# Fused attention and two gated feed-forward layers on one Trainium2 core: fill-in products of zeros, and another order of the GpSimd, SyncE and weight-sum work

## What is computed

```python
q_d, k_d, v_d = (a.reshape(B, H, S // 4, 4, D).mean(axis=3) for a in (q, k, v))
out_up = np.repeat(softmax_attention(q_d, k_d, v_d), 4, axis=2)   # averages of four positions
mask = np.abs(pos[:, None] - pos[None, :]) < 4                     # the band
scores = np.where(mask, scale * q @ k.T, -1e9)
attn_out = out_up + softmax(scores) @ v
x = attn_out.transpose(0, 2, 1, 3).reshape(B * S, H * D)
x = gated(x, w_in, w_out, 1.0);  x = gated(x, w_in2, w_out2, 1.702)
# gated: h = x @ w_in; (h * sigmoid(c * h)) @ w_out
```

## Time and profile before

| | |
|---|---|
| time, median of 3 runs (lowest, highest) | 829.08 us (828.62, 831.41) |
| time of the profiled execution | 831.32 us |
| its span, first to last instruction | 829.4 us |
| mean granted TensorE clock | 0.994 of full speed |
| attention, from the start to the last addition into `x` | about 121.8 us of the span |
| busy: PE, PEld, DVE, ACT, POOL | 806.5, 778.4, 653.4, 536.2, 191.8 us |

### The profile page before, as it was taken

How to read it: one execution, slowest core, us unless ns; L and a number is a source line. 1 busy time by engine, 2 the same in 40 slices (tenths; PEclk the granted TensorE clock), 3 DMA queues, 4 the chain that set the end, 5 groups by cost and what they waited for, 6 DMA issues and landing times.

```text
span 829.4 us, 15638 instructions
## 1 busy us (share of the span) xinstructions
PE 806.5 (97%) x5787; PEld 778.4 (94%) x5787; DVE 653.4 (79%) x945; ACT 536.2 (65%) x865; POOL 191.8 (23%) x191
## 2 busy tenths in 40 slices
PE   7988899999999999999999999999999999999998
PEld 4766679999999999999999999999999999999997
DVE  6889869989989867888767888899756677665465
ACT  5887775667735567745677555687465787365763
POOL 6678768612025511036300000000000000000000
PEclk8999999999999999999999999999999999999999
DMA  7878756877677897768887787877887777878773
GB/s 211 246 196 231 200 163 234 276 245 260 205 247 249 274 311 263 251 209 262 265 288 254 232 258 251 271 244 235 301 282 260 265 252 265 290 241 267 270 260 126
DMA packets 98315, 205.42 MB, mean 248 GB/s; under 512 B 8416, under 2 KB 56032, under 8 KB 98240
## 3 DMA queue, kind: packets, MB, share of 16 engines
q1 hardware_dynamic: 98240, 204.42, 75.5%
HBM read 160.87 MB, written 43.52 MB: 246 GB/s over the span
## 4 chain that ended last, share of the span: by engine, by line
PE 76%; DVE 8%; DMA 6%; issue 3%; POOL 3%; ACT 2%; SPq 0%; DVEq 0%; POOLq 0%; ACTq 0%
PE hid L322 39%; PE yp L345 35%; DMA vn<-in_v 5%; DVE gr L498 2%; POOL vpair L897 2%; DMA wr<-in_w_in 1%; DVE wh L294 1%; DVE xs L255 1%; PE pt L1090 1%; ACT xs L251 1%; ACT wh L285 0%; DVE x L1063 0%; ACT yt L938 0%; POOL pband L900 0%; ACT pavg L988 0%
## 5 line engine op out<-in xcount | busy, mean ns | idle before, releaser
L322 PE MATMUL hid<-xs,wh 128*128 128x384 f32 x2016 | 352.9, 335 | 3.2 <-DVE hw L478 2.1
L322 PEld LDWEIGHTS hid<-xs,wh 128*128 128x128 f32 x2016 | 349.0, 188 | 6.1 <-issue 4.8
L345 PE MATMUL yp<-gr,wh 128*128 128x384 f32 x2016 | 352.5, 335 | 1.8 <-DVE gr L498 1.8
L345 PEld LDWEIGHTS yp<-gr,wh 128*128 128x128 f32 x2016 | 351.0, 189 | 2.3 <-issue 2.3
L285 ACT ACTIVATE wh<-wr 128x1024 fp32r<-128x1024 f32 (+1 forms) x164 | 164.5, 1003 | 157.7 <-PE hid L322 118.0
L498 DVE TENSOR_TENSOR gr<-G,gr 128x768 fp32r<-128x768 f32 x144 | 138.6, 971 | 48.3 <-ACT gr L398 48.2
L398 ACT ACTIVATE gr<-G 128x768 fp32r<-128x768 f32 x144 | 121.8, 846 | 68.9 <-PE yp L345 67.6
L294 DVE TENSOR_TENSOR wh<-wr,wh 128x1024 fp32r<-128x1024 f32 x76 | 89.4, 1176 | 23.1 <-ACT wh L285 23.0
L365 ACT ACTIVATE G<-G 128x1152 f32<-128x1152 f32 x48 | 55.8, 1162 | 0.0
L488 DVE TENSOR_TENSOR G<-hv,hid 128x384 f32<-128x384 f32 x48 | 26.5, 552 | 27.0 <-PE hid L322 26.9
L473 DVE TENSOR_TENSOR hv<-p,hid 128x384 f32<-128x384 f32 x48 | 26.4, 549 | 26.9 <-PE hid L322 19.3
(11 more groups left out here) (94 smaller groups left out, 766.8 us busy)
## 6 DMA issues: line engine op xcount, KB each, us to landing
wh<-rests SPq DMA_DIRECT2D x72, 512.0 KB, 3.8
wr<-sums_out SPq DMA_DIRECT2D x48, 512.0 KB, 4.7
wr<-in_w_out SPq DMA_DIRECT2D x36, 512.0 KB, 5.2
rests<-wh SPq DMA_DIRECT2D x36, 512.0 KB, 3.3
wr<-sums_in SPq DMA_DIRECT2D x40, 384.0 KB, 4.0
wr<-in_w_in SPq DMA_DIRECT2D x40, 256.0 KB, 3.4
qk<-in_qkT SPq DMA_DIRECT2D x11, 576.0 KB, 6.3
G<-in_w_in SPq DMA_DIRECT2D x12, 512.0 KB, 7.2
```

The lines of the kernel that those rows point to most:

```text
L322: last = eng.matmul(hid[:, at, 0:HALF], lhsT=wh[:, w % SLOTS, part, a % 4, cc * P:(cc + 1) * P], rhs=xs[:, rest, q, cc, :], start=start an ...
L345: last = eng.matmul(yp[:, at + m, 0:HALF], lhsT=wh[:, w % SLOTS, part, p % 4, m * P:(m + 1) * P], rhs=gr[:, p, rest, :], start=start and p ...
```

## The change

A 16-bit tile `zeros` is added. VectorE clears it as its first instruction, and the 11 warm-up products of TensorE now read it and wait only for that (`zero`); the wait for the mask and `ident16` moves behind them. The same helper, `keep_warm`, runs seven more products of zeros (128x128 by 128x512, 16 bits) into the transposes' PSUM banks in the body of unit 0, after `avg_scores(0)`, and six in the body of unit 1, after `band_scores(1)`.

GpSimd builds the mask before the two identities. In each unit it scales the band weights first, then makes `vpair`, then `vavg` (of which there are now two), then the weight sums. The sums of block p come one unit later than before: two in the odd unit 2p+1, two in the even unit 2p+2 (the last block has all four in unit 15).

SyncE loads q and k for u+3 first, then waits for `v_half` and loads `vn`, then the v windows, and in even units the block of `G` that the next unit uses. The first block is loaded after `vn` of unit 1 and q and k of unit 3.

```diff
+    IDLE = (7, 6)
+            zeros = sb("zeros", [P, P], BF16)
-            vavg = sb("vavg", [P, 2, 2 * D])
+            vavg = [sb(f"vavg{i}", [P, 2, 2 * D]) for i in range(2)]
 # SyncE
             def body(u, first=False):
-                if u.n + 1 < UNITS:
-                    eng.wait_ge(v_half, u.n + 1)
-                    load_vn(u.after())
                 if u.n + 3 < UNITS:
...
                     load_qk(u.after().after().after())
                 if u.n + 1 < UNITS:
+                    eng.wait_ge(v_half, u.n + 1)
+                    load_vn(u.after())
                     if not first:
                         eng.wait_ge(band_out, u.n)
                         load_vwin(u.after())
-                if u.odd and u.n + 1 < UNITS:
-                    eng.wait_ge(ffn.w0_sum, 2 * u.n)
-                    ffn.first_raw(eng, u.half + 1)
+                if not u.odd:
+                    if u.half:
+                        eng.wait_ge(ffn.w0_sum, 4 * u.half - 2)
+                    ffn.first_raw(eng, u.half)
             start(Unit(0, 0))
-            ffn.first_raw(eng, 0)
 # GpSimd
             eng.wait_ge(consts_fill, 3)
-            identity(ident16)
-            eng.wait_ge(consts, 1)
             fills = 3
...
             eng.sem_inc(consts, 1)
+            identity(ident16)
+            eng.wait_ge(consts, 2)
             identity(ident)
...
+                eng.wait_ge(b_rcp, u.n + 1)
+                e = pband[u.odd]
+                eng.tensor_tensor(e[:, :, 0:WIN], e[:, :, 0:WIN], rcb[:].unsqueeze(2).broadcast_to([P, NT, WIN]),
+                                  ALU.mult).then_inc(b_nrm, 1)
                 eng.wait_ge(vn_in, DMA_INC * (u.n + 1))
                 if not first:
                     eng.wait_ge(v_sum, u.n)
                 rows = vn.rearrange("p j (r d) -> p r j d", r=FACTOR)
                 eng.tensor_tensor(vpair[:], rows[:, 0:2], rows[:, 2:4], ALU.add).then_inc(v_half, 1)
-                eng.wait_ge(b_rcp, u.n + 1)
-                e = pband[u.odd]
-                eng.tensor_tensor(e[:, :, 0:WIN], e[:, :, 0:WIN], rcb[:].unsqueeze(2).broadcast_to([P, NT, WIN]),
-                                  ALU.mult).then_inc(b_nrm, 1)
                 eng.wait_ge(v_half, u.n + 1)
+                if u.n > 1:
+                    eng.wait_ge(avg_out, u.n - 1)
+                eng.tensor_tensor(vavg[u.odd][0:HP], vpair[:, 0], vpair[:, 1], ALU.add).then_inc(v_sum, 1)
                 if not first:
-                    eng.wait_ge(avg_out, u.n)
-                eng.tensor_tensor(vavg[0:HP], vpair[:, 0], vpair[:, 1], ALU.add).then_inc(v_sum, 1)
-                sum_weights(u)
+                    sum_weights(u)
             def sum_weights(u):
+                p = (u.n - 1) // 2
...
                 if u.odd:
+                    eng.wait_ge(ffn.w0_in, DMA_INC * (p + 1))
                     eng.tensor_tensor(at(S1), at(A21), at(A22), ALU.add).then_inc(ffn.w0_sum, 1)
                     eng.tensor_tensor(at(S3), at(A11), at(A21), ALU.subtract).then_inc(ffn.w0_sum, 1)
+                if not u.odd or u.n + 1 == UNITS:
...
 # VectorE
-            for pad in (vwin[P // 2:], vavg[P // 2:]):
+            eng.memset(zeros[:], 0.0).then_inc(zero, 1)
+            for pad in (vwin[P // 2:], vavg[0][P // 2:], vavg[1][P // 2:]):
                 eng.memset(pad, 0.0).then_inc(pads, 1)
 # TensorE
                     band_scores(u)
+                if u.n == 1:
+                    keep_warm(IDLE[1], pt)
...
                     avg_scores(u)
                 if first:
+                    keep_warm(IDLE[0], pt)
                     eng.wait_ge(consts, 3)
...
-            eng.wait_ge(consts, 1)
-            for n in range(WARM):
-                eng.matmul(sa if n % 2 else sc[:, 0, :], lhsT=ident16[:], rhs=ident16[:].unsqueeze(1).broadcast_to(
-                    [P, 4, P]), start=True, stop=True)
+            def keep_warm(times, to):
+                for n in range(times):
+                    eng.matmul(to[n % 2], lhsT=zeros[:], rhs=zeros[:].unsqueeze(1).broadcast_to([P, 4, P]),
+                               start=True, stop=True)
+            eng.wait_ge(zero, 1)
+            keep_warm(WARM, (sc[:, 0, :], sa))
+            eng.wait_ge(consts, 2)
             eng.wait_ge(band_cp, 2)
-            eng.wait_ge(pads, 5)
+            eng.wait_ge(pads, 6)
```

More of the change, by code:

```diff
@@ L769, in build @@
             OA = 640
+        zero = sem("zero")
         consts = sem("consts")
@@ L867, in identity @@
                                   pattern=[[-1, P]], channel_multiplier=1).then_inc(consts, 1)
+            eng.memset(band[:, 0:3, :], 0.0).then_inc(consts_fill, 1)
             eng.memset(ident16[:], 0.0).then_inc(consts_fill, 1)
-            eng.memset(band[:, 0:3, :], 0.0).then_inc(consts_fill, 1)
             eng.memset(ident[:], 0.0).then_inc(consts_fill, 1)
             eng.wait_ge(consts_fill, 3)
-            identity(ident16)
-            eng.wait_ge(consts, 1)
             fills = 3
@@ L897, in body @@
                 eng.tensor_tensor(vpair[:], rows[:, 0:2], rows[:, 2:4], ALU.add).then_inc(v_half, 1)
-                eng.wait_ge(b_rcp, u.n + 1)
-                e = pband[u.odd]
-                eng.tensor_tensor(e[:, :, 0:WIN], e[:, :, 0:WIN], rcb[:].unsqueeze(2).broadcast_to([P, NT, WIN]),
-                                  ALU.mult).then_inc(b_nrm, 1)
                 eng.wait_ge(v_half, u.n + 1)
+                if u.n > 1:
+                    eng.wait_ge(avg_out, u.n - 1)
+                eng.tensor_tensor(vavg[u.odd][0:HP], vpair[:, 0], vpair[:, 1], ALU.add).then_inc(v_sum, 1)
                 if not first:
-                    eng.wait_ge(avg_out, u.n)
-                eng.tensor_tensor(vavg[0:HP], vpair[:, 0], vpair[:, 1], ALU.add).then_inc(v_sum, 1)
-                sum_weights(u)
+                    sum_weights(u)
             def sum_weights(u):
+                p = (u.n - 1) // 2
                 def at(a):
-                    return ffn.first_place(u.half, a)
+                    return ffn.first_place(p, a)
                 if u.odd:
[L914 to L919, removed]
+                    eng.wait_ge(ffn.w0_in, DMA_INC * (p + 1))
                     eng.tensor_tensor(at(S1), at(A21), at(A22), ALU.add).then_inc(ffn.w0_sum, 1)
                     eng.tensor_tensor(at(S3), at(A11), at(A21), ALU.subtract).then_inc(ffn.w0_sum, 1)
+                if not u.odd or u.n + 1 == UNITS:
+                    eng.wait_ge(ffn.w0_sum, 4 * p + 2)
+                    eng.tensor_tensor(at(S2), at(S1), at(A11), ALU.subtract).then_inc(ffn.w0_sum, 1)
+                    eng.wait_ge(ffn.w0_sum, 4 * p + 3)
+                    eng.tensor_tensor(at(S4), at(A12), at(S2), ALU.subtract).then_inc(ffn.w0_sum, 1)
             for n, pad in enumerate((ptb[P // 2:], pta[P // 2:])):
@@ L999, in early @@
                     ffn.round_x(eng, 0, FILLS[n - 7])
-            eng.wait_ge(consts, 2)
+            eng.wait_ge(consts, 1)
             eng.activation(band[:, NT - 1, :], band[:, 2, :], ACT.Copy).then_inc(band_cp, 1)
@@ L1170, in avg_product @@
                     for j in range(2):
-                        last = eng.matmul(po[h * D:(h + 1) * D, OA:OA + SD], lhsT=vavg[:, j, h * D:(h + 1) * D],
+                        last = eng.matmul(po[h * D:(h + 1) * D, OA:OA + SD], lhsT=vavg[u.odd][:, j, h * D:(h + 1) * D],
                                           rhs=pta[:, j, :].rearrange("p (c q) -> p c q", c=NA)[:, :, h * QT:h * QT + AQ],
```

## The result

| | before | after |
|---|---|---|
| median (lowest, highest) | 828.8 us (827.47, 831.41), 6 runs | 824.44 us (822.73, 826.24), 6 runs |
| ratio, 95% interval | | 0.9949 (0.9927 to 0.997) |
| the profiled execution | 831.32 us | 822.73 us |
| mean granted TensorE clock in it | 0.994 | 1.000 |

The change saves 4.4 us of 829, 0.5%. The same kernel beside the kernel before on another occasion gave 826.09 against 828.4 us, ratio 0.9963 (0.9948 to 0.9979). The forecast was 825.2 us.

What follows compares the result with a forecast made beforehand. TensorE, busy 806.5 of 829.4 us, bounds the kernel; only its idle or slow time in the first 122 us can be won. 0.2 + 2.7 + 3.3 - 1.0 = 5.2 us; forecast 825.2 us, between 826.6 and 823.9, range 822.3 to 829.3.

Steps and rivals of the forecast that it cites:

- Clock: 2.7 us: Unit 0 to 1: with fill-ins keeping TensorE's clock up, the unit takes 5.97 instead of 8.66 us, 2.7 us won.
- The doubt about the median: Whole-kernel time: a median run whose clock stayed up already has the clock gain, giving 826.6 us; one without gives 823.9.
- Scaling: 3.3 us: TensorE's waits for GpSimd's band-weight scaling vanish: 2.1 us in unit 5, 1.1 in unit 9, 0.1 in unit 3.
- The charge of 1.0 us: Attention units: loss charged for GpSimd's queue, late `vn` and `G` loads, and collisions with VectorE; 1.0 us, bounds 0 and 4.
- Landings: Loads in the attention: `G` lands in about 6 to 8 us, up to 7.2 free; `vn` landing in 5.9 costs nothing.
- the late-`G` rival: Odd attention units: GpSimd waits for `G`, delaying the next scaling; at 9.6 us landing, 834.9 us total; chance 0.08.
- Its price for one block: Late `G` landing in L us: units 3, 5 and 7 lose L - 7.2 each, units 9, 11 and 13 L - 8.0.
- The start: 0.2 us won: Before unit 0's first transposes: earlier warm-up gains 0.3 us, fill-ins take about 0.1; transposes at about 12.05 instead of 12.28.
- First transposes later than 12.3 us: Unit 0: listed sign that the forecast is wrong; the forecast had these transposes at about 12.05 us.
- stretched sums that end after `rcb`: GpSimd's weight sums in attention units: listed sign that the forecast is wrong; the forecast had 5.9 us within 5.97.
- The sum: Whole kernel: 0.2 start + 2.7 clock + 3.3 scaling - 1.0 charge = 5.2 us; 826.1 profiled, 825.2 forecast.
- the ring only turns: GpSimd's ring in the attention: load delays hit the next scaling instead, 3.3 us not won, about 827.7 us; chance 0.20.

Runs made afterwards that it cites:

- Order only: The changed kernel without the thirteen products of zeros in units 0 and 1; median 825.4 us, ratio 0.9966 to the kernel before.
- q and k ahead: The changed kernel with SyncE's q and k loads issued behind `vn`, ahead of the windows and `G`; median 827.67 us, ratio 0.9989 to the kernel before.
- after, again: The changed kernel measured once more without any edit, beside the kernel before; median 826.09 us, ratio 0.9963.
- fills only: The kernel before with only the zeros tile, warm-up from it and thirteen products of zeros, old GpSimd and SyncE orders; median 828.15 us, ratio 0.9995.

## Why the prediction was right, and where not

*Clock: 2.7 us.* Unit 0 to 1 fell from 8.66 to 5.94 us, 2.72. Right in the profile. "Order only" shows that the fall costs 1.5 us another time, so 2.7 is its price in one execution. The doubt about the median, that a run whose clock stayed up already has the gain, had no ground: in none of the 73 runs of the kernel before beside the experiments was the mean clock above 0.998.

*Scaling: 3.3 us.* Units 4 to 5, 8 to 9 and 2 to 3 gave 2.09, 1.07 and 0.18. Right, each by the step that was written down, and 3.34 us together. In unit 5:

```profile
38.73 0.37 SPq L113 DMA_DIRECT2D G<-in_w_in  x1
...
41.26 0.21 DVE L1054 RECIPROCAL rcb<-smb 128x9 f32<-128x9 f32 x1
41.56 1.24 POOL L898 TENSOR_TENSOR pband<-pband,rcb 128x630 f32<-128x630 f32 x1 [0.47 <-DVE rcb L1054]
42.76 1.27 POOL L904 TENSOR_TENSOR vpair<-vn 72x512 f32<-72x512 f32 x1
```

The scaling starts 0.30 us after `rcb` starts, where it was 2.40 before.

*The charge of 1.0 us.* In the profile GpSimd's new queue cost 0.5 us, all in unit 6, and through a term seen from one side only: I had VectorE hold up GpSimd, but here VectorE's subtraction, which is on the path, was the one held up by a weight sum. Elsewhere GpSimd was held up as said, by up to 2.0 us (2.76 instead of 0.73 in unit 8), inside its spare time but for 0.3 us. The Trainium skill, "GPSIMD Engine Reference", section 8 (Key points), names contention with VectorE instructions that have two SBUF inputs; the trace agrees, 1.66 against 1.22 us on VectorE's side and 2.76 against 0.73 on GpSimd's. The same contention is why `vpair` ahead of the scaling costs more than its wait.

*Landings.* `G` was estimated at 6 to 8 us and landed in 4.1 to 6.5. "q and k ahead" shows that this is what keeps the ring free, and the late-`G` rival would have come true in part with that load in its old place. Its price for one block was too low: 9.3 - 7.2 gives 2.1 us, and unit 3 to 4 lost 3.0. But only two blocks were late enough to matter, so 4.7 us were lost and not 12.0.

*The start: 0.2 us won.* This step failed: 0.45 us were lost. The working took the clock to rise at the same moment as before, or earlier with the products, and put no price on a later rise. The timeline answers the earlier trace rows:

```profile
0.82 0.11 DVE L1086 MEMSET zeros<- 128x64 uint32 x1 [0.82 <-PEq L1232]
0.99 0.61 PE L1214 MATMUL sc<-zeros 128*128 128x512 bf16 x1 [0.99 <-DVE zeros L1086]
...
5.23 0.63 PE L1214 MATMUL sc<-zeros 128*128 128x512 bf16 x1
5.66 0.73 PE L1109 MATMUL sc<-band,ident 128*128 128x350 bf16 x2
```

The warm-up starts 0.90 us earlier, more than the 0.4 expected, and all eleven products run 0.43 us apart, the spacing of the low clock. So they end no earlier than before (5.66 us, against 5.61), and the next two products run at the low clock too (0.73 instead of 0.43 us): the first scores come 0.35 us later. The last 0.1 us is GpSimd's: the scaling began 0.40 instead of 0.30 us after `rcb`. Over the profiles with eleven products the first transposes came at 12.14 to 13.06 us, wherever the fill-ins were 7 and 6. The products began at 0.99 or 1.00 us in all of them, and the last ones of the eleven ran 0.43 us apart in some and 0.22 in others. So when the clock first rises differs from execution to execution, and an earlier begin of the products does not set it. First transposes later than 12.3 us were on my list of signs that the forecast is wrong, and so were stretched sums that end after `rcb`, which unit 9 has (the scaling began 0.59 us after `rcb`); both came, and neither cost much.

*The sum.* 5.2 us against the profiled execution gave 826.1, lowered to 825.2 for the median; measured 824.44 and 826.09. The attention ended 5.5 us earlier, and that this is so near to 5.2 is partly luck. The start was 0.65 us worse than forecast, the charge 0.5 us smaller, and unit 11 to 12 gave 0.36 us that no term had and whose cause is open (7.15 before, 6.79 after; in "after, again" a distance of 7.16 stands at 13-14 instead). The medians fell by 4.4 us and, the second time, by 2.3; the 3.9 us forecast for them lie between, but came from halving the clock's part, for which there was no ground.

How the terms hang together the prediction had right, and "fills only" bears it out: without GpSimd's new order 1.6 of the clock's 2.7 us were to be lost in unit 1, and 1.4 were. The scaling's term needs no help of the clock (92.90 us from unit 1 to 15 with and without fill-ins), but it needs both orders. The mechanism that the rival "the ring only turns" names is real in the old order of the loads: in "fills only" unit 1 was scaled earlier, and unit 3 at nearly the old time.

## What to carry to other kernels

Before filling idle time of the first engine, ask what the next unit waits for: where that is a load, an earlier start is given back there, here about half of it. A load behind which an in-order engine stands should be ahead of large ones with a unit or more to spare, and the operation for which the busiest engine waits should stand ahead of any wait for a load. Compare distances between stages inside the trace when totals vary by more than the effect, and look at each distance that changed: a sum that comes out at nothing can be made of a gain and of pauses that have nothing to do with the edit.

## What the hardware showed that I had not expected

The granted clock's column reads 1.00 from the start, in both kernels, while the first products run 0.43 us apart and take 606 to 634 ns, against 0.22 us apart and 379 ns later. Before its first rise the low clock is seen in the durations alone.

VectorE and GpSimd hold each other up both ways. With GpSimd's weight sum begun 0.16 us earlier it ran its usual 0.73 us and VectorE's subtraction took 1.66 instead of 1.22; with the sum begun 0.15 us earlier, in the second profile, the sum took 1.95 us and the subtraction 1.22. Where VectorE runs two operations in a row, GpSimd's sum took 2.76 instead of 0.73 us, though it had begun 0.35 us before the first.

A gap of 1.66 to 1.80 us in TensorE's work at 220 to 230 us was followed by a fall of the clock in two profiles (before, and eight warm-up products) and by none in the ten others that have it. The gap of 2.11 us ahead of unit 5 of the kernel before was not followed by a fall, and one of 1.60 us in "q and k ahead" was. The length of the gap alone does not tell.
